# Expert tiles taken from two streams in turn, in an order computed on the chip

## The reference

```
attn_out = attention with a bucket mask on q, k, v        # 2 x 8 heads, 768 tokens, 64
x = rational MLP of attn_out as [1536, 512]               # 512 -> 2048 -> 512
logits = x @ w_gate                                       # [1536, 8]
expert_idx = argmax(logits, axis=1)
gate_w = softmax(logits)[expert_idx]
for e in range(8):                                        # w1 [8,512,1024], w2 [8,1024,512]
    mask = expert_idx == e
    out[mask] = gate_w[mask] * (relu(x[mask] @ w1[e]) @ w2[e])
```

## Time and profile before

| | before |
|---|---|
| median of 3 runs | 871.96 us (871.07 to 872.41) |
| the profiled execution | 869.42 us |
| its span, first to last instruction | 867.3 us |
| mean granted TensorE clock | 0.956 |

### The profile page before, as it was taken

One profiled execution on the slowest core, in us unless ns is written; L12 is line 12 of the kernel. 1 busy time (PEld: TensorE's weight loads), 2 busy tenths in 40 slices (PEclk: granted clock), 3 DMA queues, 4 the chain that ended last, 5 costly groups with the idle time before them and its releaser, 6 DMA issues.

```text
span 867.3 us, 12938 instructions
## 1 busy us (share of the span) xinstructions
PE 784.7 (90%) x4222; PEld 694.3 (80%) x4222; DVE 563.0 (65%) x951; ACT 489.0 (56%) x971; POOL 454.0 (52%) x402
## 2 busy tenths in 40 slices
PE   3699999999998799999999999958849999999955
PEld 2588999989997699999999998856748888888844
DVE  3378878878895788788778778944324545454521
ACT  2378778778887987788788777633323001201130
POOL 2331663464247776477477445259897201622696
PEclk8799999999999999999999999968969999999979
DMA  7598777875841932901960050557644400341322
GB/s 180 125 220 212 169 171 182 188 178 132 204 146 35 317 106 81 359 24 58 348 205 1 0 194 1 177 177 230 219 149 167 136 25 23 106 140 26 142 65 108
DMA packets 71839, 124.12 MB, mean 143 GB/s; under 512 B 33406, under 2 KB 35934, under 8 KB 67680
## 3 DMA queue, kind: packets, MB, share of 16 engines
q1 hardware_dynamic: 64272, 91.44, 38.3%
q10 hardware_dynamic: 5024, 25.56, 8.9%
q0 software_dynamic: 2480, 6.31, 1.9%
HBM read 60.21 MB, written 33.45 MB: 108 GB/s over the span
## 4 chain that ended last, share of the span: by engine, by line
PE 78%; POOL 9%; ACT 4%; DVE 3%; issue 2%; SPq 2%; DMA 1%; ACTq 0%; POOLq 0%
POOL split L726 7%; PE ps L1262 6%; PE ps L1351 5%; PE ps L1352 5%; PE ps L1350 5%; PE ps L1334 5%; PE ps L1336 5%; PE ps L1335 5%; PE ps L1475 4%; PE ps L1274 4%; PE ps L1476 4%; PE ps L1477 4%; PE ps L1253 4%; PE ps L1252 4%; PE ps L1501 3%; PE ps L1499 3%
## 5 line engine op out<-in xcount | busy, mean ns | idle before, releaser
L726 POOL TENSOR_TENSOR split<-wraw,split 128x512 fp32r<-128x512 f32 x112 | 139.4, 1283 | 109.7 <-ACT split L871 109.7
L871 ACT ACTIVATE split<-wraw 128x512 fp32r<-128x512 f32 x128 | 68.5, 617 | 199.8 <-PE ps L1477 127.5
L1018 DVE TENSOR_TENSOR ptl<-ps,pth 128x512 fp32r<-128x512 f32 x144 | 98.9, 687 | 36.3 <-ACT pth L809 34.3
L703 POOL TENSOR_TENSOR hw<-hw,ha 128x384 f32<-128x384 f32 x64 | 65.2, 1019 | 77.2 <-ACT hw L883 77.2
L809 ACT ACTIVATE pth<-ps 128x512 fp32r<-128x512 f32 x144 | 86.7, 602 | 31.2 <-PE ps L1262 31.0
L998 DVE TENSOR_REDUCE negmax<-ps 128x1 f32<-128x768 f32 x96 | 91.2, 950 | 14.8 <-PE ps L1253 14.8
L1262 PE MATMUL ps<-cst,pr 128*128 128x128 f32 x576 | 88.0, 273 | 1.5 <-ACT pr L800 1.5
L800 ACT ACTIVATE pr<-ps,negmax 128x768 f32<-128x768 f32 x96 | 86.8, 904 | 3.2 <-DVE negmax L998 3.2
L1334 PE MATMUL ps<-xh,wih 128*128 128x384 f32 x256 | 86.7, 339 | 2.0 <-DVE hp L1052 2.0
L1475 PE MATMUL ps<-split,xth 128*128 (+1 forms) x152 | 65.0, 427 | 25.4 <-POOL split L726 23.2
L1336 PE MATMUL ps<-xh,wil 128*128 128x384 f32 x256 | 86.3, 337 | 0.0
(11 more groups left out here) (160 smaller groups left out, 2022.4 us busy)
## 6 DMA issues: line engine op xcount, KB each, us to landing
routed<-blank SPq DMA_DIRECT2D x32, 771.0 KB, 14.5
wraw<-in_moe_w ACTq DMA_DIRECT2D x24, 1024.0 KB, 5.5
wraw<-in_moe_w SPq DMA_DIRECT2D x8, 1024.0 KB, 5.9
operand<-qk_hi SPq DMA_DIRECT2D x16, 384.0 KB, 4.0
operand<-qk_lo SPq DMA_DIRECT2D x32, 192.0 KB, 4.1
operand<-qk_hi SPq DMA_DIRECT2D x32, 192.0 KB, 4.3
operand<-mask SPq DMA_DIRECT2D x16, 384.0 KB, 4.8
xg<-routed SPq DMA_DIRECT2D x19, 256.0 KB, 2.6
```

What stands on the lines that cost most here:

```text
L726: pool.tensor_tensor(split_piece(E_LO[x], r % 2, k), wraw[:, x, i, :], split_piece(E_HI[x], r % 2, k).bitcast(F32), ALU.subtract).then_inc ...
```

## The change

The experts are dealt to two streams: experts 0 to 3 use slot 0, experts 4 to 7 use slot 1, each stream in the order of its experts. Every expert's tiles are cut into runs of two (48 possible runs, 6 for an expert; a run has 0, 1 or 2 tiles). Tiles are taken a run from the first stream, a run from the second, and so on; when one stream is at its end the rest of the other follows. Rounds of weights go by the first tile of each expert in that order. The first two are known beforehand, experts 0 and 4; which experts the others are, and their slots, is computed with the table. Round r now waits for the end of the expert before it in the same stream. As before, every expert has at least one tile. `routed` gets three tiles that stay blank.

The table is now computed by DVE and PE in turn, on 48 partitions, one for each possible run: 4 DVE instructions, 4 products, 7 DVE, 2 products, 4 DVE beside them, 2 products, 4 DVE, then the place and slot tables (`rows_done`, for SP), 1 DVE, 4 products, and 4 DVE to `table_done`. PE does its products ahead of the transposes of tile 0.

ACT makes the high parts of round 1 without waiting for the table. For later rounds it reads the expert and the slot into registers, and addresses the DMAs and the high parts by them; POOL reads the slot too, for its low parts.

```
-NROUTED = E * REGION
+NROUTED = E * REGION + 3
+BLANK_TILE = E * REGION
+STREAM = E // 2
+RUN = 2
+NRUN = REGION // RUN
+NSEG = E * NRUN
...
-        BLANKS = [0, 24, 54, NROUTED]
+        BLANKS = [0, 24, 57, NROUTED]
...
-                    load_weights(sp, x, 1, c)
+                    load_weights(sp, x, 1, c, STREAM)
...
+                sp.dma_start(seg[:, :], consts[:, C_SEG:C_SEG + G_END]).then_inc(s_seg, 16)
...
             rows_in(0)
-            sp.wait_ge(table_done, 1)
+            sp.wait_ge(rows_done, 1)
...
             pool.wait_ge(table_done, 1)
             for r in range(1, E):
-                weights_lo(0, r, range(8))
-                weights_lo(1, r, range(8))
+                ring = RING_STEP if r == 1 else pool.value_load(tab_place[0:1, r:r + 1], ...)
+                weights_lo(0, r, ring, range(8))
+                weights_lo(1, r, ring, range(8))
...
+            act.wait_ge(y_ready, 3 * NSTEP)
+            for x in range(2):
+                weights_hi(x, 1, RING_STEP, range(8))
             act.wait_ge(table_done, 1)
-            for r in range(1, E):
+            for r in range(2, E):
+                expert = act.value_load(tab_expert[0:1, r:r + 1], min_val=0, max_val=E - 1)
                 for x in range(2):
-                    if r == 1:
-                        act.wait_ge(y_ready, 3 * NSTEP)
-                    else:
-                        tab, used = ((tab_half, mm1_done), (tab_end, mm2_done))[x]
-                        act.wait_ge(used, act.value_load(tab[0:1, r - 2:r - 1], ...))
-                    weights_hi(x, r, range(8))
-                if r + 1 < E:
-                    for x in range(2):
-                        for c in range(2):
-                            load_weights(act, x, r + 1, c)
+                    for c in range(2):
+                        load_weights(act, x, r, c, expert)
+                ring = act.value_load(tab_place[0:1, r:r + 1], ...)
+                for x in range(2):
+                    freed, used = ((tab_half, mm1_done), (tab_end, mm2_done))[x]
+                    act.wait_ge(used, act.value_load(freed[0:1, r:r + 1], ...))
+                    weights_hi(x, r, ring, range(8))
```

The table on DVE (15 linked instructions go, these come; `on` is 48 partitions), and its products on PE:

```
+            dve.wait_ge(s_seg, 16)
+            link(dve.tensor_tensor(picked[on, :], ps[on, 3, 12 * E:13 * E], own(G_PICK, E), ALU.mult))
+            link(dve.tensor_reduce(upto[on, :], picked[on, :], AX.X, ALU.add))
+            link(dve.tensor_scalar(runs[on, 0:1], upto[on, :], own(G_ONE), None, ALU.is_gt))
+            dve.scalar_tensor_tensor(out=runs[on, 1:2], ...).then_inc(seg_dve, 1)
+            dve.wait_ge(seg_pe, 1)
...
+            link(dve.tensor_scalar(turns[on, :], ps[on, 7, 0:1], own(G_SECOND), None, ALU.add))
+            link(dve.tensor_tensor(turns[on, :], ps[on, 7, 2:3], turns[on, :], ALU.min))
...
+            dve.tensor_tensor(span[on, 1:2], span[on, 0:1], runs[on, 1:2], ALU.add).then_inc(seg_dve, 1)
...
+            link(dve.tensor_scalar(tab_rows[0:1, :], ps[0:1, 7, 192:192 + NTAB], float(BLANK_TILE), None, ALU.add))
+            dve.tensor_copy(tab_ring[0:1, :], ps[0:1, 7, 224:224 + NTAB]).then_inc(rows_done, 1)
+            dve.tensor_scalar(chosen[on, :], ..., ALU.is_equal, ALU.mult).then_inc(seg_dve, 1)
+            dve.wait_ge(seg_pe, 4)
+            link(dve.tensor_scalar(tab_need[0:1, :], ps[0:1, 7, 256:256 + NTAB], 8.0, 8.0, ALU.mult, ALU.max))
...
+            dve.tensor_scalar(tab_half[0:1, :], ..., 2.0, None, ALU.mult).then_inc(table_done, 1)

+            pe.wait_ge(seg_dve, 1)
+            pe.matmul(ps[on, 7, 0:2], seg[on, G_AHEAD:G_AHEAD + NSEG], runs[on, :], start=True, stop=True)
+            pe.matmul(ps[on, 7, 2:3], seg[on, G_OTHER:G_OTHER + NSEG], runs[on, 0:1], start=True, stop=True)
+            pe.matmul(ps[on, 7, 64:64 + NSEG], spread(runs[on, 0:1]), seg[on, G_AHEAD:G_AHEAD + NSEG], ...)
+            pe.matmul(ps[on, 7, 128:128 + NSEG], spread(runs[on, 1:2]), cst[on, C_ID:C_ID + NSEG], ...).then_inc(seg_pe, 1)
+            pe.wait_ge(seg_dve, 2)
...
+            pe.wait_ge(seg_dve, 4)
...
+            pe.matmul(ps[0:1, 7, 320:320 + E], order[on, 1:2], chosen[on, :], ...).then_inc(seg_pe, 1)
```

More of the change, by code:

```diff
@@ L74, in constants @@
     for e in range(E):
-        c[:, C_MULT + e * REGION:C_MULT + (e + 1) * REGION] = NTOK * e + P * np.arange(REGION)
-        c[:, C_MULT + e * REGION] = -1.0
         c[0, C_BASE + e] = NTOK * e
-    c[:, C_ALT:C_ALT + E - 1] = 1.0 - 2.0 * (np.arange(E - 1) % 2)
+    seg = c[0:NSEG, C_SEG:]
+    expert, run = np.arange(NSEG) // NRUN, np.arange(NSEG) % NRUN
+    stream = expert // STREAM
+    seg[np.arange(NSEG), G_PICK + expert] = 1.0
+    seg[:, G_ONE] = np.where(run == 0, -1.0, NTOK * expert + RUN * P * run)
+    seg[:, G_TWO] = NTOK * expert + RUN * P * run + P
+    seg[:, G_SECOND] = stream
+    seg[:, G_PLACE] = REGION * expert + RUN * run - BLANK_TILE
+    seg[:, G_RING] = RING_STEP * stream
+    seg[:, G_EXPERT] = expert
+    seg[:, G_LEAD] = run == 0
+    same = stream[:, None] == stream[None, :]
+    ahead = same & (np.arange(NSEG)[:, None] < np.arange(NSEG)[None, :])
+    seg[:, G_AHEAD:G_BEHIND] = ahead
+    seg[:, G_BEHIND:G_OTHER] = ahead.T
+    seg[:, G_OTHER:G_LEADS] = ~same
+    seg[:, G_LEADS:G_END] = run == 0
     c[:, C_TILE:C_TILE + NTAB] = np.arange(NTAB)
@@ L115, in build @@
         ident = cst[:, C_ID:C_ID + P]
-        table_at = put.at
+        tab = put("tab", [P, 3 * NTAB + 4 * E], I32)
+        tab_rows, tab_ring, tab_need = [tab[:, i * NTAB:(i + 1) * NTAB] for i in range(3)]
+        tab_split = tab[:, 3 * NTAB:3 * NTAB + 2 * E]
+        tab_expert, tab_place, tab_end, tab_half = [tab[:, 3 * NTAB + i * E:3 * NTAB + (i + 1) * E] for i in range(4)]
+        csel_at = put.at
         csel = put("csel", [P, 2 * P], F32)
@@ L208, in build @@
         slot = put("slot", [P, NJ], I32)
[L209 to L222, removed]
+        picked = put("picked", [P, E], F32)
+        upto = put("upto", [P, 1], F32)
+        runs = put("runs", [P, 2], F32)
+        span = put("span", [P, 2], F32)
+        turns = put("turns", [P, 1], F32)
+        passed = put("passed", [P, 1], F32)
+        sizes = put("sizes", [P, NSEG], F32)
+        passing = put("passing", [P, NSEG], F32)
+        behind = put("behind", [P, NSEG], F32)
+        inside = put("inside", [P, NTAB], F32)
+        placed = put("placed", [P, NTAB], F32)
+        shift = put("shift", [P, 1], F32)
+        order = put("order", [P, 2], F32)
+        chosen = put("chosen", [P, E], F32)
+        put = Map(csel_at)
+        seg = put("seg", [P, G_END], F32)
+        assert put.at <= csel_at + 2 * P * 4
         put = Map(expert_at)
@@ L314, in build @@
         table_done = sem("table_done")
+        rows_done = sem("rows_done")
+        seg_dve = sem("seg_dve")
+        seg_pe = sem("seg_pe")
+        s_seg = sem("s_seg")
         slot_done = sem("slot_done")
@@ L719, in _, with weights_lo @@
             g_lo(pool, NSTEP * M4 - 1)
-            def weights_lo(x, r, pieces):
+            def weights_lo(x, r, ring, pieces):
                 for i in pieces:
@@ L1153, in _ @@
[L1153 to L1157, removed]
@@ new lines, in _, with own @@
+            on = slice(0, NSEG)
+            def own(col, n=1):
+                return seg[on, col:col + n]
+            tiles = cst[on, C_TILE:C_TILE + NTAB]
+            link(dve.tensor_tensor(picked[on, :], ps[on, 3, 12 * E:13 * E], own(G_PICK, E), ALU.mult))
+            link(dve.tensor_reduce(upto[on, :], picked[on, :], AX.X, ALU.add))
+            link(dve.tensor_scalar(runs[on, 0:1], upto[on, :], own(G_ONE), None, ALU.is_gt))
+            dve.scalar_tensor_tensor(out=runs[on, 1:2], in0=upto[on, :], scalar=own(G_TWO), in1=runs[on, 0:1], op0=ALU.is_gt, op1=ALU.add).then_inc(seg_dve, 1)
@@ new lines, in _ @@
+            link(dve.tensor_tensor(span[on, 0:1], ps[on, 7, 1:2], passed[on, :], ALU.add))
+            dve.tensor_tensor(span[on, 1:2], span[on, 0:1], runs[on, 1:2], ALU.add).then_inc(seg_dve, 1)
+            dve.wait_ge(seg_dve, 2)
+            link(dve.tensor_scalar(inside[on, :], tiles, span[on, 0:1], None, ALU.is_ge))
+            link(dve.scalar_tensor_tensor(out=inside[on, :], in0=tiles, scalar=span[on, 1:2], in1=inside[on, :], op0=ALU.is_lt, op1=ALU.mult))
+            link(dve.tensor_scalar(shift[on, :], span[on, 0:1], -1.0, own(G_PLACE), ALU.mult, ALU.add))
@@ new lines, in _ @@
+            dve.scalar_tensor_tensor(out=placed[on, :], in0=tiles, scalar=shift[on, :], in1=inside[on, :], op0=ALU.add, op1=ALU.mult).then_inc(seg_dve, 1)
+            dve.wait_ge(seg_pe, 2)
+            link(dve.scalar_tensor_tensor(out=passing[on, :], in0=ps[on, 2, 128:128 + NSEG], scalar=span[on, 0:1], in1=own(G_LEADS, NSEG), op0=ALU.is_le, op1=ALU.mult))
+            link(dve.tensor_reduce(order[on, 0:1], passing[on, :], AX.X, ALU.add))
+            link(dve.tensor_tensor(behind[on, :], ps[on, 2, 192:192 + NSEG], own(G_BEHIND, NSEG), ALU.mult))
```

100 lines of the change are left out of this document (58 added, 42 removed).

## The result

| | before | after |
|---|---|---|
| median of 4 runs | 871.81 us | 918.38 us (917.81 to 919.6) |
| ratio | | 1.0537, 95% interval 1.0518 to 1.0555 |
| span of the profiled execution | 867.3 us | 917.6 us |
| mean granted clock | 0.956 | 0.940 |

A forecast was written before the change was run, and what follows sets the result against it. PE, busy 90% of the span, sets the pace; removing three waits for POOL and the slow clock saves 27.67 plus 2.81, together 30.5 us, other costs 0: 841.5 us from a median of 871.96, range 838.5 to 848.

The forecast's parts named there:

- Rounds 2 to 7: Weight rounds on ACT and POOL: each waits for the expert ahead in its stream, and W1 is ready before its tile.
- e3: Expert 3, 8 tiles, first stream, loaded in round 4: W1 ready at 677.5, first needed by tile 8 at 685.6.
- The slower rival: POOL's pieces with register addresses take over 2.1 us instead of 1.25, so POOL bounds; 905 at 1.24 extra; 4 in 100.
- The new order and the counts: Tile counts 1, 1, 1, 8, 5, 1, 1, 1; rounds 2 to 7 first needed by tiles 3, 6, 8, 10, 13, 16.
- the tightest place: Round 5, expert 5: POOL's low parts end at 708.1, tile 10 needs them at 710.2; 2.1 us spare.
- The table: The longer table on DVE and PE takes 9.6 us and ends at 586.8, 5.4 later; cost taken as 0.
- Tile 0 and tile 1 not moved: Longer table is covered, 0.5 us at tile 0 and 2.4 at mm1(1), 599.27; cost 0.
- The sum: PE from mm1(1) to mm1(18) saves 27.67 us, mm1(18) itself 2.81 more; together 30.5 us.
- The term for the slow clock behind the removed stalls: Of the 27.67 us saved on PE, 23.16 are the three stalls, the rest slow clock behind the first two.

The follow-up runs named there:

- the mended kernel: Changed kernel with one table instruction altered so that a run without tiles gets end 0 instead of its start; 838.9 us, 0.9671 of the kernel before; again 838.8, 0.9670.

## Why the prediction was wrong

**The step that failed** is in "Rounds 2 to 7": "Round 4 (e3) may overwrite slot 0 only when tile 6 is done", and with it the statement for rounds 2 to 7 that each waits for the end of the expert ahead. The code waits for the tile before the round's own. I had worked out the order from the table's formulas for the runs that have tiles, and had taken the end from what its name says. The empty runs take part in a maximum, and I didn't put them through it. Shown: with that one instruction mended, the time is 0.967 of before, where the forecast was 0.965; with it undone for either wait alone, 1.027 and 1.011; and the same wait put into the old order costs 88 us.

**The range** reached from 838.5 to 848 because no rival had a wait that is longer than the real dependence. The slower rival was POOL's pieces under register addresses. POOL's 8 pieces take 9.95 us after the change and 10.03 before, so it had no part in it. That the time came out slower, to which 5 in 100 had been given, is therefore not that rival come true.

**What else the forecast said**, by the mended kernel where the faulty wait would hide it:
- *The new order and the counts*: right. Stalls after the change stand at tiles 3, 6, 8, 10, 13 and 16, which are the first tiles of the rounds as forecast. POOL's timeline of the mended kernel, first pieces of rounds 1 to 4, and of 5, 6 and 7:

```profile
584.44 19.86 POOL L763 TENSOR_TENSOR split<-wraw,split 128x512 fp32r<-128x512 f32 x16 [3.49 <-DVE tab L1227]
606.89 20.07 POOL L763 TENSOR_TENSOR split<-wraw,split 128x512 f32 x16 [2.59 <-ACT split L909]
...
630.71 10.05 POOL L763 TENSOR_TENSOR split<-wraw,split 128x512 f32 x8 [1.31 <-ACT split L909]
...
667.74 10.06 POOL L763 TENSOR_TENSOR split<-wraw,split 128x512 f32 x8 [7.52 <-ACT split L909]
...
698.64 20.06 POOL L763 TENSOR_TENSOR split<-wraw,split 128x512 f32 x16 [1.40 <-ACT split L909]
...
721.25 10.03 POOL L763 TENSOR_TENSOR split<-wraw,split 128x512 f32 x8 [1.40 <-ACT split L909]
...
754.11 10.05 POOL L763 TENSOR_TENSOR split<-wraw,split 128x512 f32 x8 [7.52 <-ACT split L909]
```

  Forecast: 587, 609, 632, 667.5, 698, 720, 753.7. Rounds 1 and 2 are early by the shorter table. Rounds 3, 4 and 7 are set by PE: ACT waits for mm1 of tiles 3, 6 and 13 before them. Rounds 5 and 6 follow the end of POOL's round before, as the forecast had it for round 5: POOL ends at 696.09, ACT goes on at 697.72, POOL at 698.64. That is 2.55 us from round to round, where 2.4 had been put and the kernel before had 1.95. W1 of round 5 was ready at 708.7 and tile 10 started at 710.3: the tightest place held, by 1.6 us instead of 2.1.
- *The table*: the price was too high and did no harm. It took 7.3 us after the change (577.82 to 585.09), not 9.6; the first four products, on 48 partitions, take 0.84 together, where I had put 1.9 from products with 128 columns of weights.
- *Tile 0 and tile 1 not moved*: right, mm1(1) at 599.17 after the change, 599.24 in the mended kernel, 599.27 before.
- *The sum*: 30.5 us. Inside one profile, the way from mm1(1) to mm1(18) took 209.79 us in the mended kernel (599.24 to 809.03) and 237.23 before: 27.4 less, where 27.7 had been put. mm1(18) took 5.8 to its second relu instead of 8.6. The term for the slow clock behind the removed stalls was therefore no overstatement, that behind the short stall of tile 2 included. The spans of the two profiles (867.3 and 837.2) differ by 30.1, but they are of two chips; by the medians of one chip it is 28.6, both times. The missing 1.5 to 2 us of the medians I can't place; the kernel before has no profile on those chips, where it is itself 4 us faster.
- *Slow clock*, now on the other side: after the change 12 stalls of 51.9 us together come with a span 80.4 us over the mended one. The other 28.5 are 2.4 for each stall on average; tile 3's mm1, for one, takes 8.1 to its second relu instead of 5.8.

## What to carry to other kernels

A wait is priced by what its number will be, not by what it is for: put the degenerate cases (empty runs, absent experts) through the formula that makes the number, above all where it is a maximum over entries that can be empty. Such a fault only makes a kernel wait too long and leaves its output right, so it has to be looked for in the profile: stalls of one size, once a round, and a releaser that is the very last thing before the waiting work. Before an engine is let go early into a stretch in which another one has small dependent work to do, look whether they can run side by side; here a start 3 us earlier cost 19.

## What the runs showed of the hardware

**DVE held for a whole train of POOL instructions.** With POOL's 16 tensor_tensor instructions (128x512, SBUF to SBUF) back to back, one DVE instruction with two SBUF tensor inputs lasted 20.16 us instead of 0.21, and one tensor_scalar from SBUF to SBUF over 8 columns 17.68 instead of 0.27. Those with one tensor in PSUM, a reduction from SBUF, and a tensor_scalar over a single column took 0.15 to 0.26 beside the same POOL work. The Trainium skill, "SBUF — State Buffer", section "SBUF: two separate sides", says that DVE and GpSimd share a pair of ports under an exclusive lock, which a DVE instruction with two SBUF inputs, or in a two-port mode, needs, and that the loser is blocked for the winner's instruction. The kinds of instruction agree with the trace. The length doesn't: by the page an estimated wait of one piece, 1.25 us, was to be expected, and it was all that was left of 16. Whether POOL keeps the lock between its instructions or DVE loses it each time anew wasn't tested.

**A register address adds nothing to the instruction here** on ACT and POOL: 8 high parts take 4.28 us with and without, 8 low parts 9.95 and 10.03. POOL's timeline after the change, low parts of round 2:

```profile
618.30 9.95 POOL L763 TENSOR_TENSOR split<-wraw,split 128x512 f32 x8 [13.28 <-ACT split L909]
643.46 9.95 POOL L763 TENSOR_TENSOR split<-wraw,split 128x512 f32 x8 [15.21 <-ACT split L909]
```

Between rounds the mended kernel takes 0.6 us more than the kernel before (2.55 and 1.95); whether that is the reading of the registers wasn't tested.
